# Attention heads in a routed-expert kernel: another order of the per-head side work

## The chip, the cores and the metric

The kernel runs on one core of one Trainium2 chip. The metric is device time in microseconds (us) of one execution; lower is better. The core has five engines that run their own instruction streams and meet only at semaphores: TensorE (PE; matrix products), VectorE (DVE), ScalarE (ACT), GpSimd (POOL) and SyncE (SP), which here only issues DMAs.

## The reference

Three stages, float32 in and out. Only the first is touched by the change.

```python
# attention: batch 2, 8 heads, 768 positions, 64 features; proj is 64 x 6
q_bucket = sum over bits of (q @ proj > 0) * 2**bit        # likewise k_bucket
scores   = q @ k.T / 8, where q_bucket == k_bucket, else -1e9
scores  -= row maximum;  attn = exp(scores) / (row sum + 1e-9);  o = attn @ v
x = o of all heads side by side                            # 1536 tokens x 512
# dense layer: h = x @ w_in (512 x 2048); g = h if h > 0 else exp(h) - 1; y = g @ w_out
# routed layer: tokens with y @ w_skip > 0 go to their best of 8 experts
#   (relu(y @ w1[e]) @ w2[e], weighted by the gate) and are added to y
```

## The kernel before

Attention takes the first 292 us, 16 heads one after the other. To keep float32 precision in fast matrix products, each float32 value is split into a high part, rounded on ScalarE, and a low part, the rest, subtracted on VectorE or GpSimd; a product is the sum of three products of parts.

The kernel is software-pipelined over heads. In the loop over head h, TensorE does six steps s = 0 to 5, one for each tile of 128 keys. Each step has the scores of tile s (`scores`, L1181, four matmuls) and the weighted products of the tile four steps back (`weighted`, L1193, two halves of three matmuls, LAG = 4). Between them stand units of side work for later heads, in the order that `head_units` (L58) gives. Each step has three lists: what comes before the first half, between the halves, and after the second half. With a = h+1 and b = h+2 the units (`prepare`, L1152) are:
- T of b: six transposes of q and k of head b into PSUM. ScalarE rounds them (`round_qk`, L648, to `hi`), VectorE takes the rest (`low_qk`, L817, to `lo`). SyncE then copies parts of `hi` (`copy_rows`, four DMAs) and of `lo` (`copy_low_rows`, two DMAs) into the operands of head b.
- BITS of b: six matmuls with `proj`; VectorE thresholds them into bit rows of the operands (`bits`, L827, two instructions, on L835).
- MAX of a, tiles 0 to 5: two matmuls each; VectorE reduces each to a row maximum (`maximum`, L840). MAX 0 needs the bits of a and all six copies of a (L1171, L1172).
- MAX_T of a: one transpose of the maxima that `row_maxima` (L845) has gathered; VectorE writes them, negated, into an operand (`minus_maxima`, L853), which the first scores of a need.

All these, the scores too, take turns in three pairs of PSUM banks: `PSUM_ORDER` lists units in TensorE's order, unit n uses pair n % 3, and `take` (L1145) makes it wait until unit n - 3 has been consumed: T by `low_qk`, BITS by `bits`, MAX by `maximum`, MAX_T by `minus_maxima`, scores by the exponential.

Per step ScalarE takes the exponential of the scores (L671) and rounds the last one (`high_probs`, L679). The low parts of tiles 1 and 2 are subtracted on VectorE (`low_probs`, L861), those of tiles 0, 3, 4 and 5 on GpSimd (L507). Four tiles of probabilities are kept (RING). In step 3 ScalarE copies out the finished output of the head before (`outputs`, L682).

Per pair of heads the row sums travel: `load_den` brings them into a column form, `inverse_den` (L870) inverts them, `store_rden` writes them to HBM, and `load_rden` (L356) broadcasts two rows of 768 over two times 64 partitions of `rden_rows`, for GpSimd's `normalise` (L527, two products on L533). `normalise` runs in even heads from 4 on, between `low_probs` of tiles 0 and 3. At the same place GpSimd splits one tile of weights in heads 5, 7, 9 and 11 (`split_w`, L516), and a part of x in heads 13 and 15 (`split_x`, L538).

Each engine takes its stream in written order, SyncE too: a DMA that waits holds back all behind it.

Of the kernel before, what the change touches and what calls it, by code (L numbers as in the profile page):

```python
# [17 lines left out]
HEADS = B * NH  # L18
PAIRS = HEADS // 2
QT = S // P  # L20
HALF = S // 2
BITS = 6
# [23 lines left out]
EARLY = 4  # L46
# [7 lines left out]
ON_DVE = (1, 2)  # L54
# [5 lines left out]
def head_units(h, s):  # L60


    a, b = h + 1, h + 2
    plan = [[[], [("MAX", a, 0)], [("T", b, 0)]], [[], [("MAX", a, 1)], [("MAX", a, 2)]],
            [[], [("MAX", a, 3)], [("MAX", a, 4)]], [[], [("MAX", a, 5)], [("BITS", b, 0)]],
            [[("MAX_T", a, 0)], [], []], [[], [], []]][s]
    return [[x for x in part if x[1] < HEADS] for part in plan]


# [9 lines left out]
def build(nc, q, k, v, proj, w_in, w_out, w_skip, w_gate, w1, w2, out, y_rows):  # L79
    ctx = ExitStack()  # L80
    with ctx:
# [228 lines left out]
        def _(sp):  # L310
            def load_qk(h):
                if h >= 2:
                    sp.wait_ge(s_["tq_done"], h - 1)
                for i, x in enumerate((q_h, k_h)):
                    sp.dma_start(qk_nat[h % 2][:, :, i, :], x[h]).then_inc(qk_loaded[h % 2], 16)

            def load_v(h):
                if h >= 2:
                    sp.wait_ge(s_["v_ready"], h - 1)
                sp.dma_start(v_nat[h % 2][:, :, :], v_h[h]).then_inc(v_loaded[h % 2], 16)  # L320

            def load_w(j):
                if j >= W_AHEAD:
                    sp.wait_ge(s_["w_done"], j - W_AHEAD + 1)
                sp.dma_start(w_raw[j][:, 1, :].rearrange("p (c f) -> p c f", f=P), w_in_v[j]).then_inc(w_loaded[j % W_AHEAD], 16)
                sp.dma_start(w_raw[j][:, 3, :], w_out_v[j]).then_inc(w_loaded[j % W_AHEAD], 16)

            def copy_rows(h):
                i = h % 3
                if h >= 3:  # L330
                    sp.wait_ge(s_["st_done"], QT * (h - 2))
                sp.wait_ge(s_["hi_done"], h + 1)
                for dst, src in ((qb[i][0:D, :], hi[0:D, :]), (kb[i][0:D, :], hi[D:P, :]),
                                 (qa[i][D:P, :], hi[0:D, :]), (ka[i][0:D, :], hi[D:P, :])):
                    sp.dma_start(dst.bitcast(F32), src.bitcast(F32)).then_inc(rows_copied[i], 16)

            def copy_low_rows(h):
                i = h % 3
                sp.wait_ge(s_["lo_done"], h + 1)
                for dst, src in ((qa[i][0:D, :], lo[0:D, :]), (ka[i][D:P, :], lo[D:P, :])):  # L340
                    sp.dma_start(dst.bitcast(F32), src.bitcast(F32)).then_inc(rows_copied[i], 16)

            def load_den(pair):
                sp.wait_ge(s_["od_ready"], 2 * pair + 2)
                if pair:
                    sp.wait_ge(s_["rden_ready"], pair)
                for u in range(2):
                    row = D * (1 - u)
                    sp.dma_start(den[:, u, :], o_den[(2 * pair + u) % 4][row:row + 1, :]).then_inc(s_["den_loaded"], 16)

            def store_rden(pair):
                sp.wait_ge(s_["rden_ready"], pair + 1)
                for u in range(2):
                    sp.dma_start(den_rows[2 * pair + u].rearrange("(p t) -> p t", t=QT), rden[:, u * QT:(u + 1) * QT])\
                        .then_inc(s_["rden_stored"], 16)

            def load_rden(pair):
                sp.wait_ge(s_["rden_stored"], 32 * (pair + 1))
                if pair:
                    sp.wait_ge(s_["xt_ready"], pair)  # L360
                sp.dma_start(rden_rows[:, :], den_rows[2 * pair:2 * pair + 2, :].unsqueeze(1).broadcast_to([2, D, S]))\
                    .then_inc(s_["rden_loaded"], 16)
# [16 lines left out]
                    .then_inc(s_["gates_loaded"], 16)  # L379

            for h in range(HEADS):
                if h + 3 < HEADS:
                    load_qk(h + 3)
                if h + 2 < HEADS:
                    load_v(h + 2)
                    copy_rows(h + 2)
                    copy_low_rows(h + 2)
                if h % 2 and h >= 3:
                    store_rden(h // 2 - 1)
                    load_rden(h // 2 - 1)  # L390
                if h % 2 == 0 and 4 <= h < 4 + 2 * EARLY:
                    load_w(h // 2 - 2)
                if h % 2 == 0 and h:
                    load_den(h // 2 - 1)

            sp.wait_ge(s_["st_done"], QT * HEADS)
            for j in range(EARLY, EARLY + 4):
# [249 lines left out]
        def _(act):  # L647
# [9 lines left out]
            def high_of_v(h):  # L657

                u = h % 2
                at = D * u  # L660
                act.wait_ge(v_loaded[u], 16 * (h // 2 + 1))
                if h >= 2:
                    act.wait_ge(s_["pv_done"], QT * (h - 1))
                act.activation(v_hi[u][:, :, at:at + D], v_nat[u][:, :, :], ACT.Copy).then_inc(s_["v_high"], 1)
# [36 lines left out]
            for h in range(HEADS):  # L701
                for s in range(QT):
                    n = QT * h + s
                    if s == 1 and h + 2 < HEADS:
                        round_qk(h + 2)
                    exponential(n)
                    if n:
                        high_probs(n - 1)
                    if s == 3 and h:
                        outputs(h - 1)  # L710
                    if s == 5 and 0 < h < HEADS - 1:
                        high_of_v(h + 1)
# [82 lines left out]
        def _(dve):  # L795
# [21 lines left out]
            def low_qk(h):  # L817

                dve.wait_ge(s_["hi_done"], h + 1)
                if h:  # L820
                    dve.wait_ge(rows_copied[(h - 1) % 3], 96 * ((h - 1) // 3 + 1))
                    dve.wait_ge(s_["pj_done"], h)
                dve.tensor_tensor(lo[:, :].rearrange("p (b n) -> p b n", b=2), psum("T", h, 0),
                                  hi[:, :].rearrange("p (b n) -> p b n", b=2).bitcast(F32), ALU.subtract)\
                    .then_inc(s_["lo_done"], 1)
# [19 lines left out]
            def row_maxima(h):  # L845

                dve.wait_ge(s_["max_done"], QT * h + QT)
                if h:
                    dve.wait_ge(s_["mt_done"], h)
                dve.scalar_tensor_tensor(mxp[:, 0:QT], mx[:, :], -MASKED / 2, mx[:, :], ALU.is_gt, ALU.mult)\  # L850
                    .then_inc(s_["mx_ready"], 1)

            def minus_maxima(h):  # L853

                dve.wait_ge(s_["mt_done"], h + 1)
                dve.tensor_tensor(qb[h % 3][NEG_ROW:NEG_ROW + QT, :].rearrange("p (t n) -> p t n", t=QT),
                                  psum("MAX_T", h, 0)[0:QT, 0, 0:P].unsqueeze(1).broadcast_to([QT, QT, P]),
                                  diag[0:QT, :].unsqueeze(2).broadcast_to([QT, QT, P]), ALU.mult)\
                    .then_inc(s_["neg_done"], 1)

            def low_probs(n):  # L861

                dve.wait_ge(s_["p_hi_ready"], n + 1)
                if n >= RING:
                    dve.wait_ge(s_["pv_done"], n - RING + 1)
                dve.tensor_tensor(p_lo[:, n % RING, :, 0:HALF], probs[:, n % RING, :].rearrange("p (b n) -> p b n", b=2),
                                  p_hi[:, n % RING, :, 0:HALF].bitcast(F32), ALU.subtract)\
                    .then_inc(s_["p_lo_dve"], 1)

            def inverse_den(pair):  # L870

                dve.wait_ge(s_["den_loaded"], 32 * (pair + 1))
                if pair:
                    dve.wait_ge(s_["rden_stored"], 32 * pair)
                dve.reciprocal(rden[:, :], den[:, :, :].rearrange("p u t -> p (u t)")).then_inc(s_["rden_ready"], 1)
# [8 lines left out]
            bits(1)  # L884

            for h in range(HEADS):
                for t in range(QT):
                    if h + 1 < HEADS:
                        maximum(h + 1, t)
                    if t == 0 and h + 2 < HEADS:  # L890
                        low_qk(h + 2)
                    if t == 1 and h % 2 and h >= 3:
                        inverse_den(h // 2 - 1)
                if h + 1 < HEADS:
                    row_maxima(h + 1)
                low_probs(QT * h + ON_DVE[0])
                if h + 1 < HEADS:
                    minus_maxima(h + 1)
                if h + 2 < HEADS:
                    bits(h + 2)  # L900
                low_probs(QT * h + ON_DVE[1])


            for name in ("yT_ready", "lg_read", "y_stored"):
# [526 lines left out]
```

## Time and profile before

| | |
|---|---|
| time, median of 3 runs | 710.3 us (710.2 to 711.01) |
| profiled execution's own time | 710.3 us |
| its span, first to last instruction | 708.4 us |
| mean granted TensorE clock | 0.972 of 2.4 GHz |
| TensorE busy | 644.1 us, 91% of the span |
| VectorE busy | 357.1 us, 50% |
| ScalarE busy | 327.5 us, 46% |
| GpSimd busy | 244.7 us, 35% |

The profile names an instruction by its line, its engine and by output<-inputs; buffer numbers are left out. Busy TensorE time counts overlapping, pipelined matmuls, so it is no measure of work done: what counts are the stretches in which it issues nothing. A matmul of 384 columns is shown as 0.34 us long at the full clock, and the next one starts 0.18 us after it. "Idle before" an instruction is the time its engine stood still, and the name behind the arrow is what ended that.

### The profile page before, as it was taken

How to read it: one execution, taken by the hardware profiler on the slowest of the kernel's cores; microseconds unless marked ns; L12 is line 12 of the kernel's file. 1: busy time of each engine (PE TensorE's matmuls, PEld its weight loads, DVE VectorE, ACT ScalarE, POOL GpSimd, SP SyncE). 2: the span in 40 equal slices, each digit the busy share in tenths (PEclk: the TensorE clock that was granted, in tenths of full speed). 3: DMA queues.
4: the chain of work that ended last, by engine and by line, in shares of the span. 5: the costliest groups of instructions: out<-in, count | busy, mean ns of one | idle time of the engine just before them, and what ended most of it. 6: DMA issues, size and time to landing. Idle time of an engine off the chain costs nothing.

```text
span 708.4 us, 9823 instructions
## 1 busy us (share of the span) xinstructions
PE 644.1 (91%) x3632; PEld 596.8 (84%) x3632; DVE 357.1 (50%) x495; ACT 327.5 (46%) x505; POOL 244.7 (35%) x206
## 2 busy tenths in 40 slices
PE   4888888888888889999999999999999985999996
PEld 3688888888888889998999999989999965999995
DVE  6766667777776665256532223222222247546542
ACT  2356666666666667565542334233423330343330
POOL 5134466666666658923030003000004006412111
PEclk9699999999999999999999999999999985999999
DMA  7644454546463430453020002000257782899200
GB/s 171 148 106 101 101 151 104 152 109 155 103 162 100 104 94 9 142 157 104 0 90 1 1 0 86 3 0 0 83 195 255 260 299 76 303 371 330 78 11 24
DMA packets 67960, 84.00 MB, mean 119 GB/s; under 512 B 34260, under 2 KB 44500, under 8 KB 67920
## 3 DMA queue, kind: packets, MB, share of 16 engines
q1 hardware_dynamic: 66640, 79.83, 38.0%
q0 software_dynamic: 1280, 3.65, 1.6%
q8 instruction: 24, 0.39, 0.2%
q14 instruction: 16, 0.13, 0.1%
HBM read 56.64 MB, written 8.44 MB: 92 GB/s over the span
## 4 chain that ended last, share of the span: by engine, by line
PE 84%; DVE 7%; DMA 3%; issue 2%; ACT 1%; SPq 1%; POOL 0%; POOLq 0%; DVEq 0%; ACTq 0%
PE banks L1241 19%; PE banks L1252 19%; PE banks L1365 8%; PE banks L1380 6%; PE banks L1189 5%; PE banks L1190 4%; PE banks L1174 4%; PE banks L1205 4%; PE banks L1207 4%; PE banks L1206 4%; DVE k_hi_rows_T L835 2%; DVE q_hi_rows_T L835 2%; DVE row_max L843 2%; DMA y_rows<-y 2%; PE banks L1158 2%
## 5 line engine op out<-in xcount | busy, mean ns | idle before, releaser
L1241 PE MATMUL banks<-x_hi,w_split 128*128 (+1 forms) x512 | 141.7, 337 | 0.0
L512 POOL TENSOR_TENSOR probs_lo<-probs,probs_hi 128x768 fp32r<-128x768 f32 x64 | 106.8, 1688 | 68.4 <-ACT probs_hi L679 67.0
L935 DVE SCALAR_TENSOR_TENSOR g<-exp_min_h,banks 128x384 f32<-128x384 f32 x64 | 35.5, 554 | 187.8 <-ACT exp_min_h L741 187.8
L1252 PE MATMUL banks<-w_split,g_hi 128*128 128x512 f32 x384 | 120.4, 394 | 0.1
L671 ACT ACTIVATE probs<-banks 128x768 f32<-128x768 f32 x96 | 77.7, 810 | 90.2 <-PE banks L1190 90.1
L843 DVE TENSOR_REDUCE row_max<-banks 128x1 f32<-128x768 f32 x96 | 89.0, 951 | 58.2 <-PE banks L1174 58.1
L738 ACT ACTIVATE exp_min_h<-banks 128x384 f32<-128x384 f32 x64 | 31.5, 492 | 168.0 <-PE banks L1241 168.0
L1189 PE MATMUL banks<-q_lo_hi_T,k_hi_lo_T 128*128 128x384 f32 x192 | 68.7, 358 | 31.1 <-DVE k_hi_rows_T L835 31.1
L1241 PEld LDWEIGHTS banks<-x_hi,w_split 128*128 128x128 f32 x512 | 93.6, 188 | 2.7
L1241 PE MATMUL banks<-x_lo,w_split 128*128 (+1 forms) x256 | 86.0, 336 | 0.0
L1252 PEld LDWEIGHTS banks<-w_split,g_hi 128*128 128x128 f32 x384 | 70.6, 188 | 12.3 <-DVE g_lo L909 0.5
L679 ACT ACTIVATE probs_hi<-probs 128x768 fp32r<-128x768 f32 x96 | 80.5, 840 | 0.0
L1252 PE MATMUL banks<-w_split,g_lo 128*128 128x512 f32 x192 | 76.0, 396 | 0.0
L1205 PE MATMUL banks<-probs_hi,v_hi_ones 128*128 128x386 f32 x192 | 66.8, 348 | 0.9 <-ACT o_and_den L690 0.9
L1189 PEld LDWEIGHTS banks<-q_lo_hi_T,k_hi_lo_T 128*128 128x128 f32 x192 | 36.9, 192 | 35.7 <-DVE k_hi_rows_T L835 35.6
L1190 PE MATMUL banks<-q_hi_rows_T,k_hi_rows_T 128*128 128x384 f32 x192 | 65.8, 343 | 0.0
L1206 PE MATMUL banks<-probs_lo,v_hi_ones 128*128 128x386 f32 x192 | 65.5, 341 | 0.0
L1207 PE MATMUL banks<-probs_hi,v_lo_zeros 128*128 128x386 f32 x192 | 65.3, 340 | 0.0
L1365 PEld LDWEIGHTS banks<-x_T,expert_w 128*128 128x128 f32 x512 | 61.1, 199 | 1.9 <-issue 1.3
L1365 PE MATMUL banks<-x_T,expert_w 128*128 128x128 f32 x512 | 61.3, 283 | 0.9 <-DVE x_T L1053 0.9
L1174 PE MATMUL banks<-k_hi_rows_T,q_hi_rows_T 96*128 96x384 f32 x192 | 52.2, 356 | 3.4 <-DMA k_hi_lo_T<-qk_lo_T 1.2
L1241 PEld LDWEIGHTS banks<-x_lo,w_split 128*128 128x128 f32 x256 | 48.1, 188 | 2.7
(163 smaller groups left out, 1018.1 us busy)
## 6 DMA issues: line engine op xcount, KB each, us to landing
expert_w<-in_moe_w SPq DMA_DIRECT2D x32, 1024.0 KB, 6.8
w_raw<-in_moe_w_in SPq DMA_DIRECT2D x16, 256.0 KB, 4.3
w_raw<-in_moe_w_out SPq DMA_DIRECT2D x16, 256.0 KB, 5.2
qk_nat<-in_q SPq DMA_DIRECT2D x16, 192.0 KB, 3.8
qk_nat<-in_k SPq DMA_DIRECT2D x16, 192.0 KB, 4.2
v_nat<-in_v SPq DMA_DIRECT2D x16, 192.0 KB, 3.4
q_hi_rows_T<-qk_hi_T SPq DMA_DIRECT2D x16, 192.0 KB, 2.7
k_hi_rows_T<-qk_hi_T SPq DMA_DIRECT2D x16, 192.0 KB, 3.1
```

What stands on the lines that cost most here:

```text
L512: pool.tensor_tensor(p_lo[:, n % RING, :, 0:HALF], probs[:, n % RING, :].rearrange("p (b n) -> p b n", b=2), p_hi[:, n % RING, :, 0:HALF]. ...
L679: act.activation(p_hi[:, n % RING, :, 0:HALF], probs[:, n % RING, :].rearrange("p (b n) -> p b n", b=2), ACT.Copy).then_inc(s_["p_hi_ready ...
L843: dve.tensor_reduce(mx[:, t:t + 1], psum("MAX", h, t), AX.XY, ALU.max).then_inc(s_["max_done"], 1)
L1174: mm = pe.matmul(to[:, b, :], qb[h % 3][0:NEG_ROW, i * P:i * P + P], kb[h % 3][0:NEG_ROW, b * HALF:b * HALF + HALF], start=True, stop=True)
L1189: pe.matmul(to[:, b, :], ka[i][:, s * P:s * P + P], qa[i][:, half], start=True, stop=False)
L1190: mm = pe.matmul(to[:, b, :], kb[i][:, s * P:s * P + P], qb[i][:, half], start=False, stop=True)
L1205: pe.matmul(to, v_hi[h % 2][:, t, :], high, start=(t == 0), stop=False)
L1206: pe.matmul(to, v_hi[h % 2][:, t, :], low, start=False, stop=False)
L1207: mm = pe.matmul(to, v_lo[h % 2][:, t, :], high, start=False, stop=(t == QT - 1))
L1241: mm = pe.matmul(banks[:, j % 2, 0:BN], w, x, start=(c == 0 and w is hi and x is x_hi), stop=(c == KC - 1 and w is lo))
L1252: mm = pe.matmul(banks[:, 2 + t, :], g, W[:, j, part, :], start=(j == 0 and i == 0), stop=(j == FT - 1 and i == 2))
L1365: mm = pe.matmul(banks[:, j // 4, j % 4 * P:j % 4 * P + P], w1_sb[:, r, c, j * P:j * P + P], xeT[:, e % 2, c, :], start=(c == 0), stop=(c ...
```

## The change

`head_units` places the units otherwise: two MAX after each of the first three steps' scores, T at the end of step 2, MAX_T at the end of step 3, BITS directly behind the scores of step 4. ScalarE rounds q and k of head h+2 at step 3 and no longer at step 1. VectorE does all six maxima and `row_maxima` without `low_qk` between them; then `low_probs`, `low_qk`, `minus_maxima`, `low_probs`, `bits`. SyncE issues the row copies first in the loop body, then `load_den`, then the loads of q, k, v and weights, and `store_rden` and `load_rden` last. No instruction is added or removed.

```diff
@@ head_units @@
-    plan = [[[], [("MAX", a, 0)], [("T", b, 0)]], [[], [("MAX", a, 1)], [("MAX", a, 2)]],
-            [[], [("MAX", a, 3)], [("MAX", a, 4)]], [[], [("MAX", a, 5)], [("BITS", b, 0)]],
-            [[("MAX_T", a, 0)], [], []], [[], [], []]][s]
+    plan = [[[], [("MAX", a, 0)], [("MAX", a, 1)]], [[], [("MAX", a, 2)], [("MAX", a, 3)]],
+            [[], [("MAX", a, 4)], [("MAX", a, 5), ("T", b, 0)]], [[], [], [("MAX_T", a, 0)]],
+            [[("BITS", b, 0)], [], []], [[], [], []]][s]
@@ SyncE @@
             for h in range(HEADS):
+                if h + 2 < HEADS:
+                    copy_rows(h + 2)
+                if h + 2 < HEADS:
+                    copy_low_rows(h + 2)
+                if h % 2 == 0 and h:
+                    load_den(h // 2 - 1)
                 if h + 3 < HEADS:
                     load_qk(h + 3)
                 if h + 2 < HEADS:
                     load_v(h + 2)
-                    copy_rows(h + 2)
-                    copy_low_rows(h + 2)
+                if h % 2 == 0 and 4 <= h < 4 + 2 * EARLY:
+                    load_w(h // 2 - 2)
                 if h % 2 and h >= 3:
                     store_rden(h // 2 - 1)
                     load_rden(h // 2 - 1)
-                if h % 2 == 0 and 4 <= h < 4 + 2 * EARLY:
-                    load_w(h // 2 - 2)
-                if h % 2 == 0 and h:
-                    load_den(h // 2 - 1)
@@ ScalarE @@
-                    if s == 1 and h + 2 < HEADS:
+                    if s == 3 and h + 2 < HEADS:
                         round_qk(h + 2)
@@ VectorE @@
             for h in range(HEADS):
-                for t in range(QT):
-                    if h + 1 < HEADS:
+                if h + 1 < HEADS:
+                    for t in range(QT):
                         maximum(h + 1, t)
-                    if t == 0 and h + 2 < HEADS:
-                        low_qk(h + 2)
-                    if t == 1 and h % 2 and h >= 3:
-                        inverse_den(h // 2 - 1)
-                if h + 1 < HEADS:
+                        if t == 1 and h % 2 and h >= 3:
+                            inverse_den(h // 2 - 1)
                     row_maxima(h + 1)
+                elif h % 2:
+                    inverse_den(h // 2 - 1)
                 low_probs(QT * h + ON_DVE[0])
+                if h + 2 < HEADS:
+                    low_qk(h + 2)
                 if h + 1 < HEADS:
                     minus_maxima(h + 1)
+                low_probs(QT * h + ON_DVE[1])
                 if h + 2 < HEADS:
                     bits(h + 2)
-                low_probs(QT * h + ON_DVE[1])
```

## Rows read from the trace of the kernel before

**Rows 1.** The chain of work that ended last, shares of the span by engine.
```profile
PE 84%; DVE 7%; DMA 3%; issue 2%; ACT 1%; SPq 1%; POOL 0%; POOLq 0%; DVEq 0%; ACTq 0%
```
**Rows 2.** Waits, 0 to 360 us: who waited, for whom, us in total, times, longest.
```profile
PE banks L1189 <- DVE k_hi_rows_T L835: 31.1, 14, 2.3
```
**Rows 3.** Timeline of TensorE, head 9: start us, length us, instruction, idle before it.
```profile
179.49 0.34 PE L1189 MATMUL banks<-q_lo_hi_T,k_hi_lo_T 128*128 128x384 f32 x1
...
181.63 0.82 PE L1158 MATMUL banks<-ident,qk_nat 128*128 128x128 f32 x6
182.20 0.42 PE L1189 MATMUL banks<-q_lo_hi_T,k_hi_lo_T 128*128 128x384 f32 x1
...
187.26 0.34 PE L1189 MATMUL banks<-q_lo_hi_T,k_hi_lo_T 128*128 128x384 f32 x1
...
189.39 0.34 PE L1165 MATMUL banks<-qk_hi_T,proj_both_hi 128*128 128x384 f32 x1
...
192.15 0.34 PE L1207 MATMUL banks<-probs_hi,v_lo_zeros 128*128 128x384 f32 x1
194.68 0.44 PE L1189 MATMUL banks<-q_lo_hi_T,k_hi_lo_T 128*128 128x384 f32 x1 [2.19 <-DVE k_hi_rows_T L835]
...
196.54 0.34 PE L1189 MATMUL banks<-q_lo_hi_T,k_hi_lo_T 128*128 128x384 f32 x1
```
**Rows 4.** Timeline of VectorE in head 9.
```profile
189.05 0.96 DVE L843 TENSOR_REDUCE row_max<-banks 128x1 f32<-128x768 f32 x1 [0.63 <-PE banks L1174]
190.04 0.55 DVE L850 SCALAR_TENSOR_TENSOR row_max_pad<-row_max 128x6 f32<-128x6 f32 x1
190.51 0.94 DVE L866 TENSOR_TENSOR probs_lo<-probs,probs_hi 128x768 fp32r<-128x768 f32 x1
```
**Rows 5.** One line's instructions (`row_maxima`): duration ns min/median/max, first and last start.
```profile
L850 DVE SCALAR_TENSOR_TENSOR row_max_pad<-row_max x16: 166/530/1325, 21.6 to 274.6; 128x6 f32<-128x6 f32 x16
```
**Rows 6.** Timeline of ScalarE in head 9: `round_qk`.
```profile
182.48 0.82 ACT L654 ACTIVATE qk_hi_T<-banks 128x768 fp32r<-128x768 f32 x1 [0.46 <-PE banks L1158]
```
**Rows 7.** Timeline of SyncE's queue in head 9: DMA issues.
```profile
183.37 0.52 SPq L335 DMA_DIRECT2D q_hi_rows_T<-qk_hi_T  x1
...
187.16 1.21 SPq L354 DMA_DIRECT2D den_rows<-rden  x2
191.81 0.56 SPq L361 DMA_DIRECT2D rden_rows<-den_rows  x1
```
**Rows 8.** The low row copies (L341): us from issue to landing, min/median/max.
```profile
DMA to landing us min/median/max: 3.7/3.9/6.9
```
**Rows 9.** Timelines of SyncE's queue and GpSimd: the last broadcast and its user.
```profile
314.47 0.54 SPq L361 DMA_DIRECT2D rden_rows<-den_rows  x1
...
324.58 4.68 POOL L533 TENSOR_TENSOR attn_T<-o_and_den,rden_rows 64x768 f32<-64x768 f32 x2 [18.68 <-DMA rden_rows<-den_rows]
```
**Rows 10.** A stretch between them: its us, clock, DMA share, GB/s (SyncE's columns empty).
```profile
319.00:321.00 2.00, 1.00 0.13 51
```
**Rows 11.** Timeline of GpSimd, heads 9 and 10.
```profile
189.27 1.29 POOL L523 TENSOR_TENSOR w_split<-w_raw,w_split 128x512 fp32r<-128x512 f32 x1
...
198.70 4.99 POOL L512 TENSOR_TENSOR probs_lo<-probs,probs_hi 128x768 fp32r<-128x768 f32 x3
203.84 3.81 POOL L533 TENSOR_TENSOR attn_T<-o_and_den,rden_rows 64x768 f32<-64x768 f32 x2
```
**Rows 12.** Timeline of TensorE in head 14.
```profile
276.08 0.30 PE L1179 MATMUL banks<-ident,row_max_pad 128*128 128x128 f32 x1 [1.28 <-ACT probs L671]
```
**Rows 13.** Timeline of TensorE: heads 0 and 1, and the start of head 2.
```profile
26.60 0.98 PE L1174 MATMUL banks<-k_hi_rows_T,q_hi_rows_T 96*128 96x384 f32 x2 [1.02 <-issue]
...
39.71 0.44 PE L1189 MATMUL banks<-q_lo_hi_T,k_hi_lo_T 128*128 128x384 f32 x1 [2.17 <-DVE k_hi_rows_T L835]
...
42.30 0.52 PE L1189 MATMUL banks<-q_lo_hi_T,k_hi_lo_T 128*128 128x384 f32 x1
...
60.12 0.34 PE L1189 MATMUL banks<-q_lo_hi_T,k_hi_lo_T 128*128 128x384 f32 x1
```

## The prediction

> **What bounds the kernel now.** Read the chain that ended last first: 84% of it is TensorE, so only TensorE's holes and its slow stretches can give time back [rows 1]. Then the table of waits over the attention stage: one wait of TensorE stands out, 31.1 us in 14 pieces of at most 2.3 us, before the first scores matmul (L1189), released by the second half of `bits` on VectorE (L835) [rows 2]. Then TensorE's timeline of one head, to see where the hole sits. Head 9 starts at 179.49, head 10 at 196.54, so a head takes 17.05 us [rows 3]. TensorE issues without a pause until 192.15 and then stands until 194.68, when scores step 5 starts. By the three-deep ring of PSUM pairs step 5 takes the pair that BITS(h+2) used, and VectorE reaches `bits` only after six maxima, `row_maxima`, `low_probs` and `minus_maxima`. Its timeline shows that order without a gap: last maximum 189.05, `row_maxima` 190.04, `low_probs` 190.51 with 0.94, and then `minus_maxima` and the two `bits` until the matmul at 194.68 [rows 3, 4].
>
> Block costs. From 187.26 to 189.39 lie scores, both weighted halves and one MAX, 12 matmuls: 0.1775 us each [rows 3]. So scores S = 4 = 0.71, weighted W = 6 = 1.07, MAX = 2 = 0.355, BITS = 6 = 1.07. The transposes T take 0.57 (181.63 to 182.20) and make the next matmul 0.08 late. MAX_T I put at 0.1, an estimate. The hole in slots: 194.68 less 192.15 less 0.18 = 2.35.
>
> **The new order of a head**, from its first scores matmul at 0:
> - TensorE has issued 40 matmuls before MAX 5: 7.10. T starts at 7.45, scores 3 at 8.02, its W ends at 9.87, MAX_T, and scores 4 would start at 9.98. But scores 4 now takes the pair of T(h+2) and waits for `low_qk`.
> - VectorE: MAX 5 ends 0.52 after its issue (7.62), its maximum runs 7.65 to 8.61 (0.96), `row_maxima` 0.17 (its shortest [rows 5]), `low_probs` 0.94 to 9.75, `low_qk` to 10.7 (the same operation, shape and length as `low_probs`). Its other condition, `round_qk`, is done: T ends at 8.26 and ScalarE adds 0.82, as at 182.48 [rows 6].
> - So scores 4 starts at 10.75: a hole of 0.75 in place of 2.35. `minus_maxima` (to 11.7), `low_probs` (12.7) and `bits` (15.0, after BITS has ended at about 12.8) all lie before their users: scores 5 at 13.7, MAX 0 of the next head at 16.7.
>
> Head without further trouble: 17.05 - 2.35 + 0.75 = 15.45, a gain of 1.6. The hole is not gone. What is late next is `low_qk`.
>
> **SyncE's queue.** Row copies now go ahead of all else, but begin at 9.15 (after `round_qk`). Six issues take 3.8 (183.37 to 187.16), 0.63 each, so the sixth, the second low copy, starts at 12.3. The landing is 3.9 in the median [rows 7, 8]: 16.2, against 16.7 for MAX 0. So 0.5 of cover. The longest is 6.9; the weight loads, so far issued right behind the copies, now stand behind q, k and v. In odd heads the copies are followed by q, k, v (six to eight issues until 14.6), then the two stores of `store_rden`, from 14.7. In the kernel before the stores start at 187.16, which is 7.7 into the head, and the broadcast `load_rden` starts 4.65 after them, at 191.81 [rows 7]. So the broadcast moves from 12.3 to about 19.3 in the head, 7 us later, that is 3.9 into the next, even head.
>
> **The broadcast is slow.** Its last one is issued at 314.47 and releases `normalise` at 324.58: 10.1 us [rows 9]. In its second half the DMA engines' mean share is 0.13 at 51 GB/s, two engines of sixteen [rows 10]. In the kernel before, the one at 191.81 has until 203.84, when GpSimd reaches `normalise`, so it is hidden by 2 us [rows 7, 11]. It now lands 10.1 after 3.9, at about 14 of the even head, where GpSimd wants it at 7.3 (203.84 less 196.54). The Trainium skill, "DMA: Bandwidth & Descriptors", section on why a DMA increments its semaphore by 16, says the engine count is the largest number up to 16 that divides the slowest dimension of both sides; this source's is 2, and the trace agrees with two engines (share 0.13).
>
> What hangs on it, in heads 4, 6, ..., 14:
> - `normalise` 3.81 [rows 11]: 13.5 to 14, until 17.3 to 17.8. Behind it in GpSimd's order `low_probs` of tile 3, 1.67 (4.99 for three): 19.0 to 19.5. TensorE wants tile 3 in the second step of the next head, at 15.45 + 2.5 + 0.7 = 18.6. Loss 0.4 to 0.9. `low_of_v` and tile 4 then end at 21.7 to 22.2, wanted at 21.1: again 0.6 to 1.1, the same delay, not a second one.
> - The copies of the even head (9.15 to 12.9) share these two engines with the broadcast until 14. If their last share goes behind it, they land at 17 to 18 instead of 16.2, and MAX 0 waits 0.3 to 1.3. This delays the weighted products as well, so the two losses overlap. I take 1.1 for both; ends -0 and +2.6 (copies landing after 6.9 instead of 3.9, less the cover, at the slowest copy).
> - Head 14 has no T and no BITS (12.9 long), and head 15 no MAX either, so tile 3 is wanted at 12.9 + 2.5 = 15.4, while GpSimd ends it at 18 (its broadcast goes out some 1 us earlier, for head 13 has no q and k load). Loss 2.7, and 0.5 more before the first weighted product of tile 0. Against this the hole of 1.28 before MAX_T in head 14 goes [rows 12]. Net +1.8; ends -1.4 and +3.
>
> **GpSimd against VectorE.** `row_maxima` reads and writes six columns, yet takes 166 to 1325 ns [rows 5]; at 190.04 it lasted until GpSimd's instruction before it ended. That one was the last piece of the weights' split, 1.29 long, from 189.27 to 190.56 [rows 11]: the split lasts until 11.1 in an odd head, and the new `row_maxima` and `low_probs` (8.6 to 9.7) would meet it. But with the backlog from the even head GpSimd starts it at about 8.8, behind `low_probs` of VectorE, which then goes through. I charge 0.1; ends 0 and 1.2, if a piece of 1.29 of the split goes first. Beside this stands the Trainium skill, "SBUF — State Buffer", section "Who interferes with whom": a VectorE instruction with two SBUF inputs and a GpSimd one that reads SBUF exclude each other for the whole instruction. By it `low_probs` could also wait out one half of `normalise` (1.9) in the even heads, were the broadcast in time; that would make them 17.3, not 15.45.
>
> **Start.** Head 1 starts at 42.30 and head 2 at 60.12, 17.8, because the matmuls at 42.30 still take 0.52, half the clock, after the hole of 2.17 in head 0 [rows 13]. In the new head 0 MAX 0 still starts at 26.60, behind `bits`. Laid out as above, with the weighted products missing and MAX and scores at half clock up to about 31, T ends at 33.2, `low_qk` at 36.1, and head 1 starts at 40.9, an estimate: 1.4 earlier. Head 1 then is 15.45. With the slow stretch gone 3.8 in all, with it kept 2.3: I take 3.0, ends 1.5 and 3.8.
>
> **Sum** against the profiled execution's own 710.3 (span 708.4; the median of the runs is 710.3 too): start -3.0; heads 2 and 3, -3.3; heads 5, 7, 9, 11, 13 at -1.5, -7.7; heads 4 to 12 even at -0.5, -2.7; heads 14 and 15, +1.8. Together -14.9, so 695.4. The stages after attention keep their order and follow 15 us earlier. All bounds on the fast side give 686, all on the slow side 711.
>
> **Rivals.**
> - A, the broadcast costs little: it lands by 11 of the even head and the copies don't feel it. For it: in the kernel before, the copies of an even head start 8.6 us behind a broadcast (4.7 from 191.81 to the head's start, and 3.9, as 183.37 stands to 179.49), and the median landing is still 3.9. Against: its measured 10.1. Even heads then gain 1.6, the end 1.4: 695.4 - 5.5 - 3.2 = 687. Chance 0.17.
> - B, both new neighbours bite: copies of the even heads 2.6 late in MAX 0, odd heads lose 0.8 to the split. 695.4 + 5 x 1.5 + 5 x 0.7 = 706, from 701 on. Chance 0.17.
> - C, slower: the broadcast lands not 10 but 14 us after its issue, since q, k and v are still moving when it goes out. Tile 3 then is 4.4 late in five heads and 7 in head 14: +29 against the 22 that the other heads and the hole give: about 717. It decides from 13 us on: there tile 3's delay in every even head eats all gains. Chance 0.06.
> - D, the change doesn't do what it says: `low_qk` reaches scores 4 as late as `bits` reached scores 5, because VectorE's maxima wait for MAX pairs still in use. Then within 0.2%, 709 to 711.5. Against: the maxima 0 to 4 end at least 0.3 before their pair is taken again. Chance 0.04.
>
> The forecast has 0.56. Range: 689 to 702, which takes in part of A and of B. What this kernel's measurement can tell from no change is about 0.2%, 1.4 us: faster 0.90, same 0.04, slower 0.06.
>
> **What would show it.** In the changed kernel: the hole before L1189 moves to scores 4, released by `qk_lo_T` (L823), some 0.6 us each in 14 heads; L835 releases none. `attn_T` (L533) waits for the broadcast in heads 4 to 14, about 6 us each. TensorE waits for `probs_lo` of GpSimd or for `k_hi_lo_T` after even heads. Clean heads take 15.4 to 15.5. It is wrong if L1174 waits for the copies in odd heads too, or if a hole over 1.5 us stays before any L1189.

## The result, and the profile after

The changed kernel takes 720.5 us (median of four runs, 718.0 to 721.5) against 710.3 (710.1 to 711.0): ratio 1.0129, 95% interval 1.0088 to 1.0171. It is slower by 1.3%, clear of 1.0; 695.4 was forecast. All 21 recorded runs of it lie between 715.5 and 725.1, a wider spread than that of the kernel before, so a difference from it is good to some 3 us. The profiled execution took 722.2, its span is 720.3, and its mean TensorE clock 0.961 of full speed (0.972 before).

The chain of work that ended last, by engine, answers to [rows 1]:
```profile
PE 73%; DMA 12%; DVE 5%; SPq 4%; issue 2%; ACT 2%; POOL 1%; POOLq 0%; DVEq 0%; ACTq 0%
```
TensorE has gone from 84% to 73%, and DMA from 3% to 12%. Which DMA, the table of waits over the attention stage shows (who waited, for whom, us in total, times, longest), against [rows 2]:
```profile
POOL attn_T L535 <- DMA rden_rows<-den_rows: 65.0, 7, 19.4
...
PE banks L1177 <- DMA k_hi_lo_T<-qk_lo_T: 18.7, 9, 3.5
...
PE banks L1192 <- DVE qk_lo_T L825: 10.6, 14, 1.6
```
The wait for `bits` (31.1 us) has gone. In its place stand the two that the prediction named: 10.6 us at scores 4 for `low_qk`, and MAX 0 for the low row copies, 18.7 us in 9. Five of these hold 15.6: 3.21, 2.87, 2.71, 3.30 and 3.48, in heads 5, 7, 9, 11 and 13. These heads' copies go out in the even head before, while that head's broadcast still moves. Here are heads 3 to 5 in TensorE's timeline (start, length, instruction, idle before it):
```profile
82.25 0.44 PE L1192 MATMUL banks<-q_lo_hi_T,k_hi_lo_T 128*128 128x384 f32 x1 [0.45 <-DVE qk_lo_T L825]
86.93 0.34 PE L1192 MATMUL banks<-q_lo_hi_T,k_hi_lo_T 128*128 128x384 f32 x1
89.62 0.58 PE L1177 MATMUL banks<-k_hi_rows_T,q_hi_rows_T 96*128 96x384 f32 x2 [1.29 <-DMA k_hi_lo_T<-qk_lo_T]
99.03 0.44 PE L1192 MATMUL banks<-q_lo_hi_T,k_hi_lo_T 128*128 128x384 f32 x1 [0.46 <-DVE qk_lo_T L825]
108.31 0.98 PE L1177 MATMUL banks<-k_hi_rows_T,q_hi_rows_T 96*128 96x384 f32 x2 [3.21 <-DMA k_hi_lo_T<-qk_lo_T]
109.09 0.52 PE L1208 MATMUL banks<-probs_hi,v_hi_ones 128*128 128x384 f32 x1
...
113.89 0.34 PE L1209 MATMUL banks<-probs_lo,v_hi_ones 128*128 128x384 f32 x1
121.34 0.45 PE L1192 MATMUL banks<-q_lo_hi_T,k_hi_lo_T 128*128 128x384 f32 x1 [1.58 <-DVE qk_lo_T L825]
136.60 0.44 PE L1192 MATMUL banks<-q_lo_hi_T,k_hi_lo_T 128*128 128x384 f32 x1 [0.46 <-DVE qk_lo_T L825]
```
From scores 4 to scores 4 it is 15.26 us where nothing else waits (121.34 to 136.60), the 15.45 of the forecast. Across a stalled MAX 0 it is 22.31 (99.03 to 121.34). The hole is 3.21 of the 7.05 between them; scores 4 of head 5 waits 1.58 in place of 0.46, which is 1.1 more; the remaining 2.7 is in the matmuls of 0.52 behind the hole. TensorE at 109.09 runs at half its clock. The windows (us of the window, busy time and count of PE, PEld, DVE, ACT, POOL, granted clock, DMA share, GB/s):
```profile
104.00:109.00 5.00, 1.79 (x9) 1.50 (x8) 0.00 (x0) 2.23 (x4) 4.57 (x3) 0.81 0.63 147
109.00:114.00 5.00, 5.00 (x17) 5.00 (x17) 2.33 (x4) 1.54 (x2) 5.00 (x5) 0.51 0.34 108
114.00:119.00 5.00, 5.00 (x33) 4.96 (x32) 4.33 (x6) 2.64 (x4) 4.83 (x6) 1.00 0.00 0
```
17 matmuls in five busy microseconds against 33 in the next five: after the hole TensorE is at 1.2 GHz (0.51 granted) until 113.9, when it is back at 2.4. Against a head with no hole, the two steps behind the holes take 2.7, 2.9, 3.2, 3.1 and 3.0 more than the hole itself, 15.0 in all; the granted clock is 0.50 or 0.51 behind each of the five.

Why the copies are late stands in SyncE's queue and GpSimd's timeline, heads 4 and 5, against [rows 7, 9, 11]:
```profile
91.33 0.63 SPq L361 DMA_DIRECT2D rden_rows<-den_rows  x1
97.63 0.53 SPq L335 DMA_DIRECT2D q_hi_rows_T<-qk_hi_T  x1
...
101.58 0.48 SPq L341 DMA_DIRECT2D k_hi_lo_T<-qk_lo_T  x1
```
```profile
104.11 3.74 POOL L535 TENSOR_TENSOR attn_T<-o_and_den,rden_rows 64x768 f32<-64x768 f32 x2 [8.97 <-DMA rden_rows<-den_rows]
108.09 1.68 POOL L514 TENSOR_TENSOR probs_lo<-probs,probs_hi 128x768 fp32r<-128x768 f32 x1 [0.24 <-POOL attn_T L535]
...
118.31 1.30 POOL L525 TENSOR_TENSOR w_split<-w_raw,w_split 128x512 fp32r<-128x512 f32 x1
```
The broadcast leaves at 91.33, 4.4 into the even head, and `normalise` can start at 104.11, 12.8 us later. In heads 4 to 12 this takes 11.5 to 13.1 us; in head 14, which has no copies and no loads of q, k and v, 9.5 (276.96 to 286.50). The six copies go out under it, and the last, issued at 101.58, lands after 6.6 us. The table of DMAs around it, and the same around the undisturbed copy at 121.93 (KB, us to landing):
```profile
k_hi_lo_T<-qk_lo_T SPq DMA_DIRECT2D x1, 192.0 KB, 6.6
```
```profile
k_hi_lo_T<-qk_lo_T SPq DMA_DIRECT2D x1, 192.0 KB, 4.0
```
The last low copies of heads 4, 6, 8, 10 and 12 take 6.6, 6.7, 6.9, 7.1 and 7.3; those of heads 5, 7, 9 and 11 take 3.9 to 4.0. The kernel before has the same pattern. From its tables of DMAs, the last low copy of head 10, behind a broadcast, and that of head 9:
```profile
k_hi_lo_T<-qk_lo_T SPq DMA_DIRECT2D x1, 192.0 KB, 6.9
```
```profile
k_hi_lo_T<-qk_lo_T SPq DMA_DIRECT2D x1, 192.0 KB, 3.9
```
There the last low copies of heads 4, 6, 8 and 10 take 5.5, 6.2, 4.9 and 6.9, those of heads 5, 7, 9 and 11 take 3.8 or 3.9. They landed by 14 us of the head and MAX 0 wanted them at 18.3, so nothing waited. The change took that cover away.

DMA windows of the changed kernel while the broadcast moves alone, and then with the copies:
```profile
95.00:97.00 2.00, 1.00 0.13 52
97.00:99.00 2.00, 1.00 0.22 74
99.00:101.00 2.00, 1.00 1.02 238
```
0.13 is again two engines of sixteen.

All of the loss lies in the attention stage, and nearly all in heads 4 to 13 (first scores matmul of each, from TensorE's timelines):

| | before | after | difference | forecast |
|---|---|---|---|---|
| start of head 2 | 60.12 | 55.60 | -4.5 | -3.0 |
| heads 2 and 3 | 34.0 | 31.3 | -2.7 | -3.3 |
| heads 4 to 13 | 170.7 | 187.8 | +17.1 | -10.4 |
| heads 14, 15, to the next stage | 27.1 | 29.2 | +2.1 | +1.8 |
| sum | 291.9 | 303.9 | +12.0 | -14.9 |

### The profile page after: what moved, and what is told of

Its sections match the earlier page's. It is cut to its first block, busy times and chain, and to the rows that moved or that the text cites. A ratio compares the mean times of both kernels' runs of the same rounds, so it can differ in the third digit from the quotient of the medians.

```text
span 720.3 us, 9823 instructions
## 1 busy us (share of the span) xinstructions
PE 657.8 (91%) x3632; PEld 609.1 (85%) x3632; DVE 355.8 (49%) x495; ACT 327.2 (45%) x505; POOL 244.5 (34%) x206
## 4 chain that ended last, share of the span: by engine, by line
PE 73%; DMA 12%; DVE 5%; SPq 4%; issue 2%; ACT 2%; POOL 1%; POOLq 0%; DVEq 0%; ACTq 0%
PE banks L1244 19%; PE banks L1255 18%; PE banks L1368 8%; DMA k_hi_lo_T<-qk_lo_T 8%; PE banks L1383 6%; PE banks L1177 5%; SPq L335 3%; PE banks L1208 3%; PE banks L1209 3%; PE banks L1210 3%; PE banks L1192 3%; DVE row_max L845 3%; PE banks L1193 2%; DMA y_rows<-y 2%; DMA rden_rows<-den_rows 1%
## 5 line engine op out<-in xcount | busy, mean ns | idle before, releaser
L1255 PEld LDWEIGHTS banks<-w_split,g_hi 128*128 128x128 f32 x384 | 70.6, 188 | 12.3 <-DVE g_lo L912 0.5
L1192 PE MATMUL banks<-q_lo_hi_T,k_hi_lo_T 128*128 128x384 f32 x192 | 69.9, 364 | 10.6 <-DVE qk_lo_T L825 10.6
L1177 PE MATMUL banks<-k_hi_rows_T,q_hi_rows_T 96*128 96x384 f32 x192 | 57.9, 391 | 21.3 <-DMA k_hi_lo_T<-qk_lo_T 18.7
L1209 PE MATMUL banks<-probs_lo,v_hi_ones 128*128 128x386 f32 x192 | 67.6, 352 | 0.0
L1210 PE MATMUL banks<-probs_hi,v_lo_zeros 128*128 128x386 f32 x192 | 67.4, 351 | 0.0
L1177 PEld LDWEIGHTS banks<-k_hi_rows_T,q_hi_rows_T 96*128 96x128 f32 x192 | 39.8, 222 | 27.2 <-issue 24.3
L535 POOL TENSOR_TENSOR attn_T<-o_and_den,rden_rows 64x768 f32<-64x768 f32 x16 | 30.7, 1918 | 65.7 <-DMA rden_rows<-den_rows 65.0
```

The source lines that it names most:

```text
L1177: mm = pe.matmul(to[:, b, :], qb[h % 3][0:NEG_ROW, i * P:i * P + P], kb[h % 3][0:NEG_ROW, b * HALF:b * HALF + HALF], start=True, stop=True)
L1192: pe.matmul(to[:, b, :], ka[i][:, s * P:s * P + P], qa[i][:, half], start=True, stop=False)
L1209: pe.matmul(to, v_hi[h % 2][:, t, :], low, start=False, stop=False)
L1210: mm = pe.matmul(to, v_lo[h % 2][:, t, :], high, start=False, stop=(t == QT - 1))
L1255: mm = pe.matmul(banks[:, 2 + t, :], g, W[:, j, part, :], start=(j == 0 and i == 0), stop=(j == FT - 1 and i == 2))
```

## Experiments

Theory 1: the two-engine broadcast, moved into the even heads, is what costs; through the copies, and through TensorE's slow clock after each hole. Theory 2: SyncE's new order costs, since copies and q, k, v changed places. Theory 3: GpSimd, held up by `normalise`, delays the weighted products. Ratios are against the kernel before, which was run again beside each series of experiments (708.5 to 709.1); kernels of different series are compared here by their ratios.

**e1, the broadcast as two DMAs of 64 partitions each** in the changed kernel:
```
-                sp.dma_start(rden_rows[:, :], den_rows[2 * pair:2 * pair + 2, :].unsqueeze(1).broadcast_to([2, D, S]))\
-                    .then_inc(s_["rden_loaded"], 16)
+                for u in range(2):
+                    sp.dma_start(rden_rows[u * D:u * D + D, :], den_rows[2 * pair + u:2 * pair + u + 1, :].broadcast_to([D, S]))\
+                        .then_inc(s_["rden_loaded"], 16)
...
-                pool.wait_ge(s_["rden_loaded"], 16 * (pair + 1))
+                pool.wait_ge(s_["rden_loaded"], 32 * (pair + 1))
```


> The changed kernel with load_rden written as two DMAs, one for each half of 64 partitions, so that the outermost dimension of both sides is 64 and no longer 2. Theory (the broadcast on two DMA engines lies under the row copies of the even heads; they land 3 us late, and the hole of 3 us then takes the TensorE clock down): the copies of even heads land in about 4 us, the waits of 2.7 to 3.5 us before MAX 0 in heads 5 to 13 go, the clock stays up, time 691 to 698. Rival 1 (the copies are late because they are issued late, behind round_qk, with q, k, v behind them): no change, 718 to 722. Rival 2 (GpSimd's late normalise is what costs): it lands early too, so also about 695; the next run tells these apart.

Measured: 689.5 us, ratio 0.9737 (0.9692 to 0.9782), a little below the 691 expected; span 688.5. Its waits:
```profile
POOL attn_T L536 <- DMA rden_rows<-den_rows: 14.5, 3, 13.3
PE banks L1193 <- DVE qk_lo_T L826: 11.4, 14, 1.3
...
PE banks L1178 <- DMA k_hi_lo_T<-qk_lo_T: 3.5, 5, 1.1
```
13.3 of the 14.5 is the last broadcast, after attention. The low copies land in 3.9 at the median and 5.5 at most. The same bytes, issued at 123.69, move in two microseconds:
```profile
124.70:125.70 1.00, 1.00 0.52 175
125.70:126.70 1.00, 1.00 0.68 218
```
0.68 of sixteen is eleven engines' worth, against two. Heads 2 to 13 take 15.88 us each (56.81 to 247.32), where the forecast had 15.9. That these agree is luck: the forecast has 1.1 for copies in every even head, which e1 does not pay, and e1 pays 0.7 to 1.4 at scores 4 where the changed kernel pays 0.46 in clean heads. The profiled span falls by 31.8 us, and the two ratios differ by 28 (give or take 4): all that made the changed kernel slow is in this one DMA's form. The Trainium skill, "DMA: Bandwidth & Descriptors", section on why a DMA increments its semaphore by 16, takes the largest count up to 16 that divides the slowest dimension of both sides; 64 gives sixteen engines, and the trace agrees as far as eleven at least.

**e5, the same edit in the kernel before.**

> The kernel before with the broadcast as two DMAs of 64 partitions each. Theory: there it is hidden, by 2 us at GpSimd and behind the copies, so 709.5 to 711. If it also slowed something in the kernel before, a gain of 1 us or more.

Measured: 708.8, ratio 0.9994 (0.9979 to 1.0009). The time is just under the range given, but the ratio shows no change. There the slow broadcast was hidden, so its speed was worth nothing. It did slow the copies: with the split, the last low copies of heads 4, 6, 8 and 10 land in 3.8, 4.8, 3.8 and 3.9, where they took 5.5, 6.2, 4.9 and 6.9. The change is what made it cost.

**e3, in the changed kernel `store_rden` and `load_rden` moved ahead of the odd head's copies:**
```
             for h in range(HEADS):
+                if h % 2 and h >= 3:
+                    store_rden(h // 2 - 1)
+                    load_rden(h // 2 - 1)
...
-                if h % 2 and h >= 3:
-                    store_rden(h // 2 - 1)
-                    load_rden(h // 2 - 1)
```


> The changed kernel with store_rden and load_rden ahead of the row copies in odd heads. The broadcast, still on two engines, then goes out at about 9 us of the odd head, just before that head's copies, and lands by about 5 us of the even head, before GpSimd wants it at 7.3. Theory: the late copies move from the even heads to the odd ones; waits of 2 to 4 us before MAX 0 now in heads 4, 6, ..., 14, none of note in odd heads; time 708 to 722. Rival 2 (GpSimd): its wait is gone, time about 695.

Measured: 744.0, ratio 1.0503 (1.0469 to 1.0537). TensorE's timeline, head 4:
```profile
95.30 0.98 PE L1177 MATMUL banks<-k_hi_rows_T,q_hi_rows_T 96*128 96x384 f32 x2 [6.10 <-DMA k_hi_lo_T<-qk_lo_T]
```
MAX 0 waits in heads 4, 6, ..., 14 (5.8 to 6.9 each) and in no odd head from 3 on, and low copies take up to 11.3 to land. GpSimd has its broadcast in time in all of them (it waits for the last one only). So the stall follows the broadcast to whichever head's copies come behind it. The place was expected, the size was not: 6 us and not 2 to 4, and 744 and not at most 722.

**e4, the hole of MAX 0 filled** in heads 5 to 13 with 16 matmuls whose result is overwritten:
```
                         pe.wait_ge(s_["bits_done"], h + 1)
+                        if h >= 6 and h % 2 == 0:
+                            m = QT * (h - 1) - LAG
+                            for _ in range(16):
+                                pe.matmul(to[:, 0, :], v_hi[m // QT % 2][:, m % QT, :], p_hi[:, m % RING, 1, 0:HALF],
+                                          start=True, stop=True)
                         pe.wait_ge(rows_copied[h % 3], 96 * (h // 3 + 1))
```


> The changed kernel; before TensorE waits for the row copies ahead of MAX 0 in heads 5, 7, 9, 11 and 13 it does 16 matmuls of 384 columns whose result is overwritten (2.8 us at the full clock). Theory: the clock falls because of the hole; with the hole filled it stays up, each of the five heads loses only the 3 us of the wait: 706 to 711. Rival (the clock falls for another reason, or the slow stretch costs nothing): 719 to 722.

Measured: 708.65, ratio 1.0003 (0.9987 to 1.002). The granted clock in tenths over 40 slices of the span, the changed kernel and then e4:
```profile
PEclk9999998989898989999999999999999995999999
```
```profile
PEclk9999999999999999999999999999999995999999
```
In tenths, the dips that came with the holes are gone, and the copies still land late (up to 8.9). 80 more matmuls that compute nothing of use make the kernel faster: by 9 us, give or take 3, going by the two ratios, by 12.0 going by the two profiled spans. In the traces heads 4 to 13 take 10.2 us less. The filler (14.2) and what is left of the waits behind it (1.90, 1.76 and 0.34) hold TensorE 2.6 us longer than the five holes did, but of the 15.0 us that the steps behind the holes lost only 3.0 are left. Four of the five slow stretches are gone. The fifth is shorter, behind the 1.76 in head 7 (TensorE's timeline of e4):
```profile
144.79 0.62 PE L1182 MATMUL banks<-k_hi_rows_T,q_hi_rows_T 96*128 96x384 f32 x2 [1.76 <-DMA k_hi_lo_T<-qk_lo_T]
...
146.45 0.53 PE L1197 MATMUL banks<-q_lo_hi_T,k_hi_lo_T 128*128 128x384 f32 x1
```
The hole of 1.90 in head 5 has the full clock behind it and costs 0.3 more than its length. So the half clock is worth most of 3 us for each hole.

**e2 and e6, SyncE's old order** in the changed kernel, and in e1:
```
             for h in range(HEADS):
-                if h + 2 < HEADS:
-                    copy_rows(h + 2)
...
                 if h + 3 < HEADS:
                     load_qk(h + 3)
                 if h + 2 < HEADS:
                     load_v(h + 2)
+                    copy_rows(h + 2)
+                    copy_low_rows(h + 2)
```


> The changed kernel with the SyncE order of the kernel before: loads of q, k, v ahead of the row copies, stores and broadcast behind them (still on two DMA engines). The other engines keep the new order. Theory: the load of q and k waits for T at 8.3 us of the head, so the copies begin at 10 to 11 and the last is issued at about 14, lands at about 18, against 16.7 for MAX 0: a wait of 1 to 2 us in all 14 heads; the copies of even heads start later under the broadcast than in the changed kernel and are late by 2 to 4 in all. Time 710 to 735. Rival 1 (the new SyncE order is what makes the copies late): below 705.

> The same with the broadcast as two DMAs of 64 partitions. It prices the SyncE reordering alone, without the slow broadcast. Theory: the copies are still 1 to 2 us late in each head, 14 heads: 700 to 712, against 689.5 with the new SyncE order. If the reordering is worth nothing without the slow broadcast: 688 to 692.

Measured: e2 716.8, ratio 1.013 (1.0095 to 1.0166); e6 688.5, ratio 0.971 (0.9691 to 0.9729). My expectation for e6, 700 or more, missed. I had read that q and k of head h+3 wait for T of head h+2, and so would hold the copies up; they wait for T of head h+1, done a head earlier. Theory 2 falls: with the split broadcast both orders give the same time (ratios 0.9737 and 0.971, intervals overlapping), and with the slow one too (1.0129 and 1.013). For e2 the time lay in the range, but the wait that was expected in all 14 heads came in heads 5, 7, 9, 11 and 13 (1.8 to 4.7) and, under 1 us, in heads 1 and 2. In e2 the broadcast goes out at 88.17 and 126.12, only 2 to 3 us sooner, still behind the copies, which start late because `round_qk` does. So the old order of SyncE doesn't bring the broadcast back; that it is the move of T and `round_qk` that takes it along, I conclude from this and from the queue, and didn't try by itself.

**e9, GpSimd late, the copies undisturbed:** e1 with `load_rden` issued behind the even head's copies.
```
                     copy_low_rows(h + 2)
+                if h % 2 == 0 and h >= 4:
+                    load_rden(h // 2 - 2)
...
                     store_rden(h // 2 - 1)
-                    load_rden(h // 2 - 1)
+                    if h == HEADS - 1:
+                        load_rden(h // 2 - 1)
```


> The changed kernel with the broadcast as two DMAs of 64 partitions, issued behind the low row copies of the even head (at about 12.9 us of it), for heads 4 to 14. The copies are not disturbed; GpSimd gets the broadcast at about 16.5 us of the even head, as late as in the changed kernel (104.11, which is 16 us after its head's start). It separates the two things that a late broadcast does. If GpSimd's lateness costs by itself: tile 3 is done at 16.5 + 3.8 + 1.7 = 22, wanted at 18.6, so a hole of about 3 us in each of heads 5 to 15, with the slow clock behind it: 700 to 715. If the copies alone matter (rival 2 out altogether): 688 to 692.

Measured: 726.8, ratio 1.0248 (1.0223 to 1.0273). GpSimd, and then TensorE, heads 4 and 5:
```profile
106.61 3.67 POOL L539 TENSOR_TENSOR attn_T<-o_and_den,rden_rows 64x768 f32<-64x768 f32 x2 [11.65 <-DMA rden_rows<-den_rows]
110.52 1.67 POOL L518 TENSOR_TENSOR probs_lo<-probs,probs_hi 128x768 fp32r<-128x768 f32 x1 [0.24 <-POOL attn_T L539]
```
```profile
112.25 0.69 PE L1212 MATMUL banks<-probs_hi,v_hi_ones 128*128 128x386 f32 x1 [5.51 <-POOL probs_lo L518]
```
```profile
PE banks L1212 <- POOL probs_lo L518: 25.9, 5, 5.5
```
MAX 0 hardly waits for a copy (2.1 us in 3, the longest 0.9), but TensorE waits five times for GpSimd's tile 3, 25.9 us in all. Both are over the expectation of 700 to 715 with holes of 3 us: the broadcast goes out at 13.0 to 13.6 and lands at 18.0 to 19.0 of the head, not at 16.5. Against e1 this is 36 us by the ratios: 25.9 of holes and about 13 that the matmuls behind them lose, less what e9 saves at scores 4 and MAX 0. So theory 3 is a mechanism of its own: a broadcast at 106.6 is as costly as disturbed copies. In e9 TensorE asks for tile 3 at 106.7 (112.25 less 5.51). In the changed kernel `normalise` starts 2.5 us earlier, tile 3 is ready at 109.77, and TensorE, held at MAX 0 until 108.31, asks for it later than that and does not wait. The copies' hole covers GpSimd's lateness.

**e7, e10: the version the runs point to.** e1, with `low_qk` ahead of both `low_probs` on VectorE; e10 with SyncE's old order too.
```
-                low_probs(QT * h + ON_DVE[0])
                 if h + 2 < HEADS:
                     low_qk(h + 2)
                 if h + 1 < HEADS:
                     minus_maxima(h + 1)
+                low_probs(QT * h + ON_DVE[0])
                 low_probs(QT * h + ON_DVE[1])
```


> The changed kernel with the broadcast as two DMAs, and on VectorE low_qk and minus_maxima ahead of both low_probs. Theory: what holds scores 4 is VectorE's chain up to low_qk, of which low_probs is 0.95 us and is no input; the wait before L1193/L1189 (0.45 to 1.35 us in each of 14 heads) goes almost away; the head gets 0.5 to 0.8 shorter, but the last row copy then is issued at 12.3 us of a head of 14.6 and MAX 0 waits up to 1 us for it. Time 682 to 689. If the wait for T's rounding on ScalarE binds as well: 687 to 690.

> The kernel e7 (low_qk and minus_maxima first on VectorE, broadcast as two DMAs) with the SyncE order of the kernel before. With the broadcast fixed the SyncE order made no difference that could be seen (688.5 against 689.5), so none is expected here: 682 to 686. If the shorter head leaves the copies less cover, so that it matters that q, k and v are issued ahead of them: above 687.

Measured: e7 684.4, ratio 0.9664 (0.9636 to 0.9691), the lowest of all; e10 686.1, ratio 0.9675 (0.9651 to 0.97), no different from e7 within the intervals. The last hole that the prediction still charged, at scores 4, shrinks from 11.4 us in 14 to:
```profile
PE banks L1193 <- DVE qk_lo_T L826: 3.1, 7, 0.8
```

**e8, two of the four high copies issued by ScalarE** behind `round_qk`, in e7:
```
+                    if n < 2 or h < 2:
+                        sp.dma_start(dst.bitcast(F32), src.bitcast(F32)).then_inc(rows_copied[i], 16)
...
                         round_qk(h + 2)
+                        for dst, src in ((qa[i][D:P, :], hi[0:D, :]), (ka[i][0:D, :], hi[D:P, :])):
+                            act.dma_start(dst.bitcast(F32), src.bitcast(F32)).then_inc(rows_copied[i], 16)
```


> The kernel of the run before with two of the four copies of the high parts issued from ScalarE's queue right behind round_qk. The low copies are then issued at about 10.7 and 11.3 us of the head, not 11.7 and 12.3, and land 1 us sooner. Theory: the waits before MAX 0 go below 0.3 us; ScalarE has slack for two issues: 3 to 8 us less than the run before, 678 to 684. If issuing costs ScalarE more than its slack, the exponential waits move into TensorE: no gain, or a loss.

Measured: 696.0, ratio 0.9818 (0.9795 to 0.984), 11.6 slower than e7: the other outcome named, a loss. ScalarE's timeline:
```profile
115.86 0.48 ACTq L715 DMA_DIRECT2D q_lo_hi_T<-qk_hi_T  x1
116.37 0.62 ACTq L715 DMA_DIRECT2D k_hi_lo_T<-qk_hi_T  x1
117.09 0.81 ACT L675 ACTIVATE probs<-banks 128x768 f32<-128x768 f32 x1 [1.31 <-issue]
```
Each head, ScalarE's next `exponential` starts up to 1.7 us late (20.6 us in 14), and TensorE then waits for ScalarE, where e7 waits 1.8 us in 2 before the weighted products and not at all before BITS:
```profile
PE banks L1216 <- ACT o_and_den L694: 8.1, 15, 1.0
PE banks L1176 <- ACT probs L675: 3.8, 12, 0.5
```
That costs more than taking two issues (0.6 each) out of SyncE's queue brings: MAX 0 waits 2.1 us for copies, against 3.1 in e7.

## Why the prediction was wrong

- *The clean head, 15.45.* Right: 15.26. The holes moved to scores 4, 0.46 where 0.75 was put, and no hole is left before scores 5.
- *The broadcast moves 7 us, to 3.9 in the even head, and takes 10.1.* Right in place (2.2 to 4.4), low in length: 11.5 to 13.1. Head 14's, with no copies under it, took 9.5, so what moves beside the broadcast slows it too; which of the copies and loads does, no run parts.
- *Even heads lose 1.1 by copies and GpSimd together.* **The step that failed.** "They land at 17 to 18 instead of 16.2, and MAX 0 waits 0.3 to 1.3" assumed that they end soon after the broadcast. They landed in 6.6 to 7.3, and MAX 0 waited 2.7 to 3.5: 15.6 us in five, where 5.5 was charged (in heads 6, 10 and 12 the last copy was also issued at 12.7 of the head, not 12.3). The rows were there: the longest landing in [rows 8], 6.9, is no stray value but a copy behind a broadcast, and with 0.5 of cover it gives 2.5 and more. I kept it as the far end of the range, and took the median of 3.9, over heads with and without a broadcast before them, as a sign that the copies are not slowed. The landings by head say the opposite, and e5 confirms them.
- *No term for the clock after a new hole.* The second failure, an omission. [Rows 13] had the pattern, matmuls of 0.52 behind a hole, and I used it for the start only. The steps behind the five holes lost 15.0 us; e4, which keeps the clock up behind four of them, is 9 to 12 us faster.
- *Odd heads lose 0.1 to GpSimd's split of the weights.* Mis-sized. Scores 4 in heads 5, 7, 9 and 11 waits 1.58, 1.33, 1.07 and 1.09 in place of 0.46, 3.2 in all. In heads 7, 9 and 11 it is `row_maxima` that is held (1.06, 0.81 and 0.81 in place of 0.17), in head 5 `low_probs`:
```profile
118.33 2.09 DVE L868 TENSOR_TENSOR probs_lo<-probs,probs_hi 128x768 fp32r<-128x768 f32 x1
```
  2.09 in place of 0.96, beside the split's piece of 118.31 to 119.61. I had let GpSimd start the split at 8.8 in the head; it had the piece under way when `low_probs` came. The Trainium skill, "SBUF — State Buffer", section "Who interferes with whom", gives the pair of ports to whichever starts first for its whole instruction; the trace agrees both ways, for in e1 `low_probs` starts at 114.00 first and GpSimd's piece of 0.62 takes 1.40.
- *Start, -3.0.* It was -4.5: the slow stretch after head 0 went, and head 1 started at 39.19, not 40.9. About 1 us of this belongs to the run and not to the change: e1, e3, e4 and e9 have the same order up to here and start head 1 at 40.15 to 40.27, and the kernel before, in e5's run, starts head 2 at 58.93, not 60.12.
- *Heads 2 and 3, -3.3.* It was -2.7: MAX 0 of head 2 waits 0.60 for a copy.
- *Heads 14 and 15, +1.8.* +2.1, but the parts differ: the waits for `probs_lo` of GpSimd are 0.76 and 0.61, 1.4 where 3.2 was charged, and the 1.28 before MAX_T that went was made up by 0.86 for ScalarE's `outputs` and 0.29 for a copy. That the sum fits is luck.
- *The sum itself* has 7.7 for five heads at 1.5 and 2.7 for five at 0.5, 0.4 too much in all, which changes nothing.
- *The rivals.* A (687) is what the kernel would be if the broadcast were cheap: e1 measured 689.5. C named the right sign and nearly the size (717), by a late tile 3; e9 shows that its mechanism exists and is dearer than priced, yet in the changed kernel it lies under the copies' hole. B added the right two effects, without the clock. The 17.3 for even heads, had the broadcast come in time, is answered by e1, where it does: heads 6, 8, 10 and 12 take 15.63, 16.22, 15.63 and 15.63. In three of them `row_maxima`, one place earlier, runs into the first half of `normalise` and is held 0.4, and `low_probs` (0.95) then goes ahead of the second half; in head 8 `row_maxima` takes 1.15.
- *The signs.* The second sign of being wrong came, narrowly: a hole of 1.58 at scores 4 of head 5. MAX 0 waited for copies issued in odd heads too, less than behind a broadcast: 0.60, 1.29 and 0.29 behind those of heads 1, 3 and 13.

In sum: heads 4 to 13 came out 27.5 us over their forecast. The holes at MAX 0 are 10.1 of it and what the steps behind them lost, nearly all of it to the half clock, 15.0; the split adds 2.7, and clean heads are 1.9 better. Head 4 adds 1.5, with its MAX 0 hole of 1.29 (e1 has it too, 1.06). These make 27.4.

## What to carry to other kernels

Before you move a DMA, look at how many engines it runs on and what will be issued behind it: a transfer on two engines that costs nothing where it is hidden (e5, no change) cost some 30 us where sixteen-engine copies with half a microsecond of cover came under it, and one more DMA instruction took that away. A median over all heads hid that copies behind the broadcast were already late in the kernel before: split such a row by what was issued ahead of it before trusting it. When a step can open a hole of some 3 us on TensorE, add the half clock behind it, here some 3 us for each, and take the longest landing of a row as the case to price where the cover is thinner than its spread. When a late resource holds up two engines, curing one path only shows the other (e9).

## What the runs showed of the hardware

- Two DMA issues in ScalarE's stream, of 0.48 and 0.62, left it idle for 1.31 before its next instruction, 0.2 more than the two together (e8).
- The holes of 2.2 us before scores 5 in the kernel before, heads 1 to 13, left the clock at full (1.00 from 60 to 270 us), those of 2.7 to 3.5 here did not. The one in head 0, no longer than the others, was followed by matmuls of 0.52 too [rows 13], and in e4 a hole of 1.76 was and one of 1.90 was not, so length alone doesn't decide.
- The last low copy landed in 10.0 to 11.3 us where the first of its six copies was issued 2.2 to 3.3 us behind a two-engine broadcast (e3), in 6.6 to 7.3 at 5.9 to 6.8 behind it (the changed kernel), in 5.4 to 8.2 at 7.8 to 8.9 (e2), and in 4.1 to 6.9 at 8.6 to 9.7 (the kernel before); with no such broadcast ahead of it, mostly in 3.7 to 4.0. The delay tends to fall as the broadcast's head start grows, but not strictly.
